# TensorE's order in a tile of attention: the three score banks ahead of the nine transposes

## The reference

```python
q_pool = q.reshape(B, H, S // 2, 2, D).mean(axis=3)
scores = scale * np.matmul(q_pool, k.transpose(0, 1, 3, 2))
attn = np.exp(scores - np.max(scores, axis=-1, keepdims=True))
attn = attn / (np.sum(attn, axis=-1, keepdims=True) + 1e-09)
out = np.matmul(attn, v)
# x: the heads side by side, 2304 x 512
h = x @ w_in;  g = np.where(h >= 1, h, np.where(h <= -1, 0, (h + 1) ** 2 / 4))
x = g @ w_out
x = np.maximum(np.maximum(x @ w1, x @ w2), x @ w3) @ w2_out
```

## Time and profile before

| | |
|---|---|
| median of 3 runs | 1314.72 us (1313.18 to 1314.82) |
| the profiled execution | 1312.52 us, of which the span of the trace is 1310.7 |
| TensorE, matmuls | busy 1264.3 us, 96% of the span |
| TensorE, weight loads | 1209.9 us, 92% |
| VectorE | 763.2 us, 58% |
| ScalarE | 659.9 us, 50% |
| GpSimd | 335.9 us, 26% |
| chain of work that ended last | PE 78%, ACT 13%, issue 5%, DVE 2% |
| granted TensorE clock | 0.993 |

### The profile page before, as it was taken

One profiled execution on the slowest core, in us unless ns is written; L12 is line 12 of the kernel. 1 busy time (PEld: TensorE's weight loads), 2 busy tenths in 40 slices (PEclk: granted clock), 3 DMA queues, 4 the chain that ended last, 5 costly groups with the idle time before them and its releaser, 6 DMA issues.

```text
span 1310.7 us, 24528 instructions
## 1 busy us (share of the span) xinstructions
PE 1264.3 (96%) x7876; PEld 1209.9 (92%) x7876; DVE 763.2 (58%) x1579; ACT 659.9 (50%) x1570; POOL 335.9 (26%) x332
## 2 busy tenths in 40 slices
PE   7999899998989999998999999999999999999998
PEld 6989898897989898988999999999999999999997
DVE  5888788787878788884544444444453223222221
ACT  5899888887979888982222222222222111111111
POOL 4244344433444443257900000000083000000000
PEclk9999999999999999999999999999999999999999
DMA  3111111111111111022400000000031000000000
GB/s 118 47 56 56 55 28 54 37 54 46 54 55 54 52 30 54 20 68 83 133 17 1 1 1 1 1 1 0 0 113 48 1 25 6 20 25 1 24 24 24
DMA packets 59119, 48.65 MB, mean 37 GB/s; under 512 B 2976, under 2 KB 48032, under 8 KB 59040
## 3 DMA queue, kind: packets, MB, share of 16 engines
q1 hardware_dynamic: 59040, 47.72, 12.2%
HBM read 42.99 MB, written 4.72 MB: 36 GB/s over the span
## 4 chain that ended last, share of the span: by engine, by line
PE 78%; ACT 13%; issue 5%; DVE 2%; POOL 1%; DMA 1%; ACTq 0%; SPq 0%; DVEq 0%; POOLq 0%
PE hid L868 32%; PE acc L900 15%; PE trans L413 8%; ACT probs L558 6%; PE acc L932 6%; PE values L475 5%; PE scores L456 5%; PE scores L458 4%; ACT pT_hi L548 3%; PE trans L424 1%; ACT value_aux L582 1%; DVE qT L662 1%; ACT qT L571 1%; ACT X L578 1%; PE trans L434 1%
## 5 line engine op out<-in xcount | busy, mean ns | idle before, releaser
L626 DVE TENSOR_REDUCE neg_max_parts<-scores 128x1 f32<-128x384 f32 x432 | 232.8, 552 | 38.5 <-PE scores L458 26.0
L640 DVE TENSOR_TENSOR pT_lo<-trans,pT_hi 128x384 fp32r<-128x384 f32 x432 | 213.3, 549 | 23.3 <-issue 16.6
L548 ACT ACTIVATE pT_hi<-trans 128x384 fp32r<-128x384 f32 x432 | 191.7, 491 | 58.7 <-PE trans L413 55.1
L558 ACT ACTIVATE probs<-scores,neg_max 128x768 f32<-128x768 f32 (+1 forms) x288 | 212.0, 753 | 4.3 <-DVE neg_max L633 4.3
L456 PE MATMUL scores<-kT,qT 128*128 128x384 f32 x480 | 201.4, 420 | 7.2 <-ACT probs L558 6.3
L413 PE MATMUL trans<-ident,probs 128*128 128x128 f32 x1296 | 192.1, 276 | 9.7 <-DVE qT L662 6.5
L413 PEld LDWEIGHTS trans<-ident,probs 128*128 128x128 f32 x1296 | 159.3, 142 | 25.9 <-issue 8.5
L868 PE MATMUL hid<-qT,w_slots 128*128 128x384 f32 x936 | 171.5, 336 | 0.0
L868 PE MATMUL hid<-x_hi,w_slots 128*128 128x384 f32 x624 | 167.6, 335 | 0.0
L868 PEld LDWEIGHTS hid<-qT,w_slots 128*128 128x128 f32 x936 | 163.7, 188 | 1.0
L458 PE MATMUL scores<-kT,qT 128*128 128x384 f32 x480 | 163.4, 340 | 0.0
(11 more groups left out here) (101 smaller groups left out, 1997.5 us busy)
## 6 DMA issues: line engine op xcount, KB each, us to landing
k_raw<-in_k SPq DMA_DIRECT2D x16, 576.0 KB, 4.7
v_raw<-in_v SPq DMA_DIRECT2D x32, 288.0 KB, 2.8
q_raw<-in_q SPq DMA_DIRECT2D x32, 256.0 KB, 2.7
out<-X SPq DMA_DIRECT2D x18, 256.0 KB, 2.6
q_raw<-in_moe_w_out SPq DMA_DIRECT2D x14, 256.0 KB, 3.0
k_raw<-in_moe_w SPq DMA_DIRECT2D x12, 256.0 KB, 3.1
k_raw<-in_moe_w_in SPq DMA_DIRECT2D x8, 256.0 KB, 2.8
k_raw<-in_moe_w_out SPq DMA_DIRECT2D x8, 256.0 KB, 2.9
```

Source lines behind the costliest of these rows:

```text
L548: act.activation(*tile_places(pT[0], src, t, g), ACT.Copy).then_inc(p_hi_done, 1)
L558: act.activation(probs[:, par, :].rearrange("p (n k) -> p n k", n=GROUPS)[:, ns[0]:ns[-1] + 1], scores[:, bank:bank + len(ns), 0:SB], ACT. ...
L626: dve.tensor_reduce(neg_max_parts[:, par, n:n + 1], scores[:, score_banks(u9)[n], 0:SB], AX_X, ALU.max, negate=True).then_inc(parts_done, 1)
L640: dve.tensor_tensor(*tile_places(pT[1], src, t, g), hi.bitcast(F32), ALU.subtract).then_inc(p_lo_done, 1)
```

## The change

One list is changed: TensorE computes S1, S2 and N0, then the nine transposes, then the products into values and the preparation. The number and the content of instructions, the buffers, the semaphores and the orders of the other engines stay. As the order of groups in the ring `trans` is made from T and X alone, it stays too.

```diff
-PE_ORDER = ["S1", "T0", "S2", "T1", "T2", "N0", "V", "X"]
+PE_ORDER = ["S1", "S2", "N0", "T0", "T1", "T2", "V", "X"]
 ACT_ORDER = ["T0", "T1", "T2", "E0", "E1", "X", "V"]
 DVE_ORDER = ["T0", "T1", "T2", "M0", "X", "M1", "M2"]
```

## The result

The changed kernel takes 1375.4 us (median of 4 runs, 1375.1 to 1377.6), the kernel before 1314.8 (4 runs). The ratio is 1.0464, with a 95% interval of 1.0446 to 1.0483: slower by 61 us, where 54 were forecast and the range ended at 1389. The profiled execution took 1375.2 us, with a span of 1373.4 against 1310.7.

What follows compares the result with a forecast made beforehand. A closed chain of exponential, scores, transposes and copies was taken to bound attention. Step times summed to 81.3 us a loop body against 74.53, +6.8, eight times +54; 1312.5 + 54 = 1366.5, median 2.2 above: 1369 us, range 1349 to 1389.

Steps and rivals of the forecast that it cites:

- The ring: Attention stage: the closed chain E0 (a tile's first exponential), scores, transposes, copies, next E0 sets the time, 3.46 us before.
- Plain steps: Steps 8 and 14: three score banks now stand between E0 and T0; 3.85 us from E0 to E0, against 3.46.
- those with N0 of the tile of both heads: Steps 2 and 11: N0 of tiles 4 and 13 has two more matmuls, 0.35 us a bank; 4.20 us.
- the single first exponential: Steps 5, 9, 13: E0 takes one bank, so S2, now ahead of T0, waits for the second exponential; 4.07 us.
- step 17: Last tile of a loop body: the first score bank also needs the second exponential; 4.42 us.
- the steps with key and value copies: Steps 4, 6, 10, 15: ScalarE's own work sets them at 3.96 us, 3.95 before, so the change costs nothing.
- The query step: Steps 7 and 16: N0's wait for the low queries now stands ahead of T0; 5.74 us, against 4.93.
- The loop's end: Steps 0 and 1: VectorE's "issue" wait hides most of the change; E0(0) to E0(2) 12.15 us, against 11.89.
- TensorE sets the pace: Rival, attention stage: the longer chain falls into TensorE's slack and fewer transpose-to-score changes help; 1300 us, faster; chance 0.04.
- The ring grows less: Rival, steps 7 and 16: low queries are early enough, taking 2 x 0.82 us from a body; +41, 1356 us; chance 0.17.
- It grows more: Rival: each score bank behind a wait costs 0.46 us, 1.38 instead of 1.16; 1401 us, or 1385 for half; chance 0.13.
- The clock: Rival: TensorE's added idle time in each tile brings the 1.2 GHz level, some 1.15 us a tile; 1534 us; chance 0.02.

Runs made afterwards that it cites:

- few_values_before: Kernel before the change, with eight of the eighteen matmuls of each group of products into values left out: 1320.0 us, ratio to before 1.0053.
- few_values_after: Changed kernel with eight of the eighteen matmuls of each group of products into values left out: 1384.3 us, ratio to before 1.0544.
- n0_twice_in_ring: Changed kernel with the matmuls of N0 done twice into the same bank, ahead of T0: 1427.7 us, ratio to before 1.0880.
- query_step_late: Changed kernel, but in steps 7 and 16 N0 stands behind T2 as before: 1362.0 us, ratio to before 1.0360.
- the unrolled kernels: Attention loops of TensorE, ScalarE and VectorE written out: 1294.6 us against the kernel before with its order, 1354.0 against the changed kernel with its order.
- t0_first: Against the kernel before, T0 moved ahead of S1, with S1, S2, T0, T1, T2, N0 in steps 7 and 16: 1311.0 us, ratio 0.9981.
- n0_ahead: Against the kernel before, only N0 moved, ahead of T1, with T0 still behind S1: 1364.1 us, ratio 1.0379.

## Why the prediction was right, point by point
**The ring.** Right, as the place of the loss and in size. Plain steps were worked out as 3.85 and came at 3.86, those with N0 of the tile of both heads 4.20 and 4.22, with its S1 and S2 4.55 and 4.58, with the single first exponential 4.07 and 4.08, step 17 4.42 and 4.43. Of the steps with key and value copies, for which 3.96 was worked out, 4 and 10 came at 3.96. They cost nothing, as forecast: ScalarE's own work had been setting them already.

Steps 6 and 15 are a miss that the table hides. They came at 3.86, below their 3.94 before. In the kernel before it wasn't ScalarE that set them: in step 6, S1 started 1.29 us behind E0 and not 1.04, behind ten products and three key transposes, with TensorE never idle, and few_values_before brings both steps to 3.79. So for these two the forecast's reason, ScalarE's own work, was wrong: it was TensorE's, beside the ring. The row came out near its forecast (0.1 for 0.3) by luck: step 4 of the first body and steps 10 and 15 of the last, which have fewer such copies, lost 0.3 to 0.4 us each.

Two independent signs that it is the ring: 67 us less of TensorE's work beside it win nothing (few_values_after), and 0.35 us more on it count in full in 16 steps of 18 (n0_twice_in_ring).

**The query step.** Right in mechanism, 0.18 us too small: 5.92 for 5.74. The term that was mis-sized is the 0.05 us that I put between the end of the low queries and N0; it took 0.24. I had the 0.05 from links between TensorE and ScalarE; why this one, behind VectorE, takes longer, no run shows. In the 15 such steps 0.18 us make 2.7, which covers the 2.4 us between 13.0 and 15.4. query_step_late shows the term by itself: 1.1 us a step. What I didn't see is that the low queries were on the ring before, too, through T0's bank of `trans`:

```profile
337.23 0.54 PE L413 MATMUL trans<-ident,probs 128*128 128x128 f32 x3 [0.40 <-DVE qT L662]
```

T0 needs one of the three low queries there, and N0 now needs all three.

**The loop's end.** Here the forecast failed in size: 2.1 us forecast for steps 0 and 1, 8.4 measured. The time after was nearly right: E0(0) to E0(2) takes 12.41 us in the mean where there is a branch, and I had 12.15. The time before was not. I read one end of the kernel before and took it for all; with 11.89 us it is the longest of five, in the mean 10.94, and the only one at the low clock from the first key transpose on. And I counted eight ends, where there are five with a branch. "This wait hides most of the change" was wrong, too: the stall grew, from a mean of 3.31 us to 4.16, and all five ends ran at the low clock behind it, where three had. The reason for the longer stall stays open; that the branch makes it, the unrolled kernels show. Of the 8.4 us, 3.7 are the ring's (0.39 us in each step 0, 0.13 in each step 1, with or without a branch), and 4.7 stand at the branches; by the spans of the unrolled kernels it is 2.4 (60.3 us between them, 62.7 with the loops). The 6.3 us between 2.1 and 8.4 and the query step's 2.4 are nearly all of the 9.2 by which the table's sum (63.2) is above the forecast's; by the medians the loss is 61, and the forecast 7 short of it.

**TensorE sets the pace** (0.04, 1300 us) fell: the kernel is slower with TensorE less busy, and taking work off TensorE made neither order faster. The Trainium skill's rule (Perfetto Trace Analysis, Identifying the Most-Contended Engine) to improve the engine of the highest occupancy would have missed this change: TensorE had the highest share in both kernels, and neither its work nor its share said what the order would do. In t0_first, where the ring is shortened instead, TensorE's work does come forward as the bound by the trace, at 3.43 to 3.50 us a tile.

**The ring grows less** (0.17) was wrong in its reason: the low queries are not early enough. **It grows more** (0.13): six score matmuls in a row take 1.15 us, not 1.38.

**The clock** (0.02, 1534 us) didn't fall between tiles. From 60 to 160 us, with TensorE idle for 8 us of 100 in short gaps, the granted clock is 1.00, that is the level of 2.4 GHz; few_values_after has 83.3 us of work in the same stretch and also 1.00. In the steps of the changed kernel the lower level shows at the loop's ends alone, behind 3.34 to 3.56 us of idle TensorE. In the kernel before it shows behind 2.59, 2.98 and 3.36 us and not behind 2.44 and 2.71, so that the idle time alone doesn't say when it comes. In few_values_after it also shows in two steps 17. In one of them TensorE, with few products to do, had been idle twice:

```profile
331.66 0.44 PE L456 MATMUL scores<-kT,qT 128*128 128x384 f32 x1 [1.02 <-DVE qT L664]
...
335.39 0.45 PE L456 MATMUL scores<-kT,qT 128*128 128x384 f32 x1 [1.87 <-ACT probs L560]
...
336.59 2.12 PE L413 MATMUL trans<-ident,probs 128*128 128x128 f32 x9
```

Nine transposes take 2.12 us there and 1.14 otherwise, the step takes 5.37 for 4.43, and the granted clock is 0.53 from 338 to 340 us. The same two gaps stand in the same place of four other bodies, at a granted clock of 1.00 behind them. So the rival's mechanism exists, but what sets it off is open. The Trainium skill (TensorE: Matmul & The Clock Gate, A second HAM failure mode: psum-queue depth-cycling) tells of something like it. With all products done, no step of the changed kernel away from the loop's ends showed it.

## What to carry to other kernels
Where several engines are all nearly busy, write down the closed chain between them, one price a link, and ask of each moved instruction whether its new place is on that chain or beside it: N0's two matmuls cost 0.35 us in a plain step on it and nothing beside it. Ask it step by step, too: here two steps of 18 were set by TensorE's own work before the change, and not by the chain or by ScalarE. A wait that comes with a moved instruction moves too; look for the few steps in which it is late, not only for the usual one. For a stall that comes once a loop body, read all its occurrences before one of them is made a term of a sum.

## What the runs showed that I had not expected
Less work made the kernel slower: with 512 matmuls of 0.13 us left out, the changed order took 1384 us for 1375, and the order of before 1320 for 1314. In the trace of the first, 2.7 us of it stand at the five loop ends and 2.5 in the steps 17, with a granted clock of 0.93 from 260 to 360 us where it is 0.97 with all the work. Another 1.1 stand in step 1 of the first body and 3.1 behind the last exponential; what makes these isn't shown.

The stall behind a loop's branch isn't a constant: VectorE's "issue" wait at the same instruction was 2.94 to 3.85 us in the kernel before, 4.04 to 4.26 after, and 4.54 to 5.10 in n0_ahead, where the step took up to 10.35 us for 3.95 without a branch. Written-out loops take all of it away: with the order of before they are 19 us faster than the kernel before and 81 us faster than the changed one.
